# Thresholds of a routing read from PSUM, and the first comparison of a layer pair cut in three

## The reference, cut to what matters

```python
def _moe_ref(x, w_gate, w1, w2):
    N, D = x.shape                    # 3072, 320
    E = w_gate.shape[1]               # 8
    cap = N // E                      # 384
    logits = x @ w_gate
    order = np.argsort(-logits.flatten())
    for idx in order:
        tok, e = (int(idx) // E, int(idx) % E)
        if assigned[tok] >= 0 or counts[e] >= cap:
            continue
        assigned[tok] = e
        counts[e] += 1
    for e in range(E):
        mask = assigned == e
        h = np.maximum(x[mask] @ w1[e], 0.0)      # 320 -> 1024
        out[mask] = h @ w2[e]                     # 1024 -> 320

def _moe2_ref(x, w_in, w_out):
    h = x @ w_in                                  # 320 -> 2048
    g = np.where(h > 0.0, h, np.exp(np.minimum(h, 0.0)) - 1.0)
    return g @ w_out                              # 2048 -> 320
```

## Time and profile before

| | us |
|---|---|
| three runs: median (lowest, highest) | 913.61 (910.56, 917.07) |
| the profiled execution, whole time | 910.03 |
| its span | 908.3 |
| mean granted clock of TensorE | 0.95 |
| PE busy | 786.0 |
| DVE, ACT, POOL busy | 573.8, 462.0, 445.2 |

### The profile page before, as it was taken

The page is one execution under the profiler, slowest core; times in us unless marked ns, Lnnn a source line. Parts: engine busy times, 40 slices in busy tenths (PEclk is TensorE's granted clock), DMA queues, the critical chain, the costliest instruction groups (busy, mean ns, idle before and its releaser), DMA issues.

```text
span 908.3 us, 18300 instructions
## 1 busy us (share of the span) xinstructions
PE 786.0 (87%) x5822; PEld 720.6 (79%) x5822; DVE 573.8 (63%) x1576; ACT 462.0 (51%) x981; POOL 445.2 (49%) x469
## 2 busy tenths in 40 slices
PE   1898999982158899989989998998999899999995
PEld 1787888882138799879969987897999789899894
DVE  7475767676855865687586567748656774643341
ACT  1444444432221775377276537826662773685573
POOL 6544444444460575186256518625661773374133
PEclk9999999996557999999999999999999999999998
DMA  4978788833321120221112022121202211121000
GB/s 68 142 126 139 125 131 131 138 71 95 116 74 42 43 65 30 63 63 45 64 43 65 26 61 70 44 66 44 65 16 64 78 45 58 47 66 37 1 1 22
DMA packets 138516, 61.04 MB, mean 67 GB/s; under 512 B 104704, under 2 KB 136704, under 8 KB 138432
## 3 DMA queue, kind: packets, MB, share of 16 engines
q1 hardware_dynamic: 136128, 52.13, 26.9%
q0 software_dynamic: 2304, 7.87, 2.7%
HBM read 51.72 MB, written 8.26 MB: 66 GB/s over the span
## 4 chain that ended last, share of the span: by engine, by line
PE 53%; DVE 11%; ACT 7%; issue 4%; POOL 2%; DMA 1%; ACTq 0%; DVEq 0%; SPq 0%; POOLq 0%
PE bank L1673 6%; PE bank L1603 6%; PE bank L1675 5%; PE bank L1674 5%; PE bank L1607 5%; PE bank L1604 5%; DVE cmp L754 3%; PE bank L1611 3%; PE bank L1609 3%; PE bank L1649 3%; PE bank L1647 3%; PE bank L1648 3%; PE bank L1632 1%; PE bank L1635 1%; ACT unit L1481 1%
## 5 line engine op out<-in xcount | busy, mean ns | idle before, releaser
L1105 POOL TENSOR_TENSOR gl_lo<-unit,gl_hi 128x384 fp32r<-128x384 f32 x128 | 142.0, 1109 | 126.3 <-ACT gl_hi L1493 125.4
L1673 PE MATMUL bank<-Wo_hi,gl_hi 128*128 128x320 f32 x384 | 126.8, 330 | 8.9 <-POOL gl_lo L1105 8.3
L1675 PE MATMUL bank<-Wo_hi,gl_lo 128*128 128x320 f32 x384 | 119.7, 312 | 0.0
L1674 PE MATMUL bank<-Wo_lo,gl_hi 128*128 128x320 f32 x384 | 119.4, 311 | 0.0
L1350 DVE SCALAR_TENSOR_TENSOR unit<-bank,unit 128x384 f32<-128x384 f32 x104 | 57.6, 554 | 90.5 <-ACT bank L1486 90.5
L1084 POOL DMA_INDIRECT xg<-x_rows,idx x24 | 26.3, 1097 | 159.3 <-DVE idx L1319 82.8
L1461 ACT ACTIVATE hid_hi<-bank 128x384 fp32r<-128x384 f32 x64 | 31.4, 490 | 136.8 <-PE bank L1611 134.4
L1478 ACT ACTIVATE unit<-bank 128x384 f32<-128x384 f32 x128 | 62.0, 484 | 66.1 <-PE bank L1611 65.9
L1603 PE MATMUL bank<-x_hi,Wi_hi 128*128 128x384 f32 x256 | 93.5, 365 | 2.0 <-DVE unit L1353 0.9
L1604 PE MATMUL bank<-x_hi,Wi_lo 128*128 128x384 f32 x256 | 86.8, 339 | 0.0
L1673 PEld LDWEIGHTS bank<-Wo_hi,gl_hi 128*128 128x128 f32 x384 | 73.1, 190 | 14.1 <-POOL gl_lo L1105 14.1
(11 more groups left out here) (252 smaller groups left out, 2143.1 us busy)
## 6 DMA issues: line engine op xcount, KB each, us to landing
stage<-in_moe_w_dram SPq DMA_DIRECT2D x32, 320.0 KB, 3.0
stage<-in_moe_w_dram SPq DMA_DIRECT2D x32, 256.0 KB, 2.6
stage<-in_moe_w_dram SPq DMA_DIRECT2D x96, 64.0 KB, 2.4
q_in<-in_q_dram SPq DMA_DIRECT2D x24, 160.0 KB, 3.3
k_in<-in_k_dram SPq DMA_DIRECT2D x24, 160.0 KB, 3.9
o_in<-in_o_gate_dram SPq DMA_DIRECT2D x24, 160.0 KB, 4.1
v_in<-in_v_dram SPq DMA_DIRECT2D x24, 160.0 KB, 4.1
x_rows<-xt SPq DMA_DIRECT2D x24, 160.0 KB, 1.8
```

The source lines that it names most:

```text
L1105: nc.gpsimd.tensor_tensor(gl_lo[:, b, :], ex[:, b, :], gl_hi[:, b, :].bitcast(F32), ALU.subtract).then_inc(gl_ok, 1)
L1673: nc.tensor.matmul(acc[j][:, 0:DM], gl_hi[:, f % RG, t_], Wo_hi[:, f, :], start=(f == 0), stop=False)
L1674: nc.tensor.matmul(acc[j][:, 0:DM], gl_hi[:, f % RG, t_], Wo_lo[:, f, :], start=False, stop=False)
L1675: ins = nc.tensor.matmul(acc[j][:, 0:DM], gl_lo[:, f % RG, t_], Wo_hi[:, f, :], start=False, stop=(f == NF2 - 1))
```

## The change

All rows of thresholds that the second stage reads are held in PSUM: the five of rounds 2 to 6 are written there at once (bank 7, columns 304 up), and ramp1 and slots are copied there (bank 7, columns 176 up; bank 6, columns 384 up) by two more instructions at the end of the mixer. The copies of ramp1 and slots in SBUF stay: the mixer reads ramp1, and later experts read slots. The first expert's one-hot blocks read slots from PSUM. pParts moves to columns 144 to 175 of bank 7.

In the six bodies the keys (choose_keys) are made with choose_start ahead of the change of layer, and the first comparison, in two halves of 12 tiles at f = 3 and 4 and ahead of the ELU, is in three parts of 8 tiles behind the ELU of f = 1, 2 and 3. For the second expert, ahead of the first body, it is in three parts as well, with the columns of the first expert between; on PE the three blocks of columns stand ahead of count_takers. In the mixer, steps of the keys move one tile earlier.

```diff
@@ RoutingTables
+        self.ramp1_p = bank[7][:, 176:176 + first_n]
+        self.ramps_p = bank[7][:, 304:304 + (len(STEPS) - 1) * 33].rearrange("p (q n) -> p q n", n=33)
+        self.slots_p = bank[6][:, 384:512]
@@ by_vector
-            nc.vector.tensor_scalar(self.ramps[:, q, 0:n], self.ramp_i[:, low:low + n],
+            nc.vector.tensor_scalar(self.ramps_p[:, q, 0:n], self.ramp_i[:, low:low + n],
                                     step * (1.0 if q + 1 < HIGH else UNIT), None, ALU.mult)
+        nc.vector.tensor_copy(self.ramp1_p, self.ramp1[:])
+        nc.vector.tensor_copy(self.slots_p, self.slots_i[:])
@@ first_compare
-            in1=self.ramp1[:, :].unsqueeze(1).broadcast_to([P, n, many]), op0=ALU.subtract, op1=ALU.is_ge)
+            in1=ramp.unsqueeze(1).broadcast_to([P, n, many]), op0=ALU.subtract, op1=ALU.is_ge)
@@ experts
-    ramps, down, slots, rows2, marks = tables.ramps, tables.down, tables.slots, tables.rows2, tables.marks
+    ramps, down, slots, rows2, marks = tables.ramps_p, tables.down, tables.slots, tables.rows2, tables.marks
-    pParts = pR[:, 192:192 + SIDE * E]
+    pParts = pR[:, 144:144 + SIDE * E]
@@ compare_first
+        SLICES = 3
         def compare_first(k, part):
-            ins = tables.first_compare(dve, *part_of(k, part), keys_at(k))
-            if part != 0:
+            n = G // SLICES
+            ins = tables.first_compare(dve, tables.ramp1_p, slice(part * n, part * n + n), n, keys_at(k))
+            if part == SLICES - 1:
                 ins.then_inc(cmp_ok, 1)
@@ choose_spots
-                ins = nc.vector.tensor_scalar(spot[:, g, :], slots[:], row[:, g:g + 1], None, ALU.is_equal)
+                ins = nc.vector.tensor_scalar(spot[:, g, :], tables.slots_p if first_expert(k) else slots[:], row[:, g:g + 1],
+                                              None, ALU.is_equal)
@@ DVE, ahead of the first body
-        compare_first(1, None)
+        compare_first(1, 0)
+        compare_first(1, 1)
         columns(0, 0)
-        round_test(1, 1)
+        compare_first(1, 2)
         columns(0, 1)
         columns(0, 2)
+        round_test(1, 1)
         round_move(1, 1)
@@ DVE, body
             if after == 2:
                 choose_start(c + 1)
+                choose_keys(c + 1)
             between_layers(k)
...
-                    if f == 2:
-                        choose_keys(c + 1)
-                    elif f == 3:
-                        compare_first(c + 1, 0)
-                    elif f == 4:
-                        compare_first(c + 1, 1)
-                    elif q >= 1 and odd:
+                    if q >= 1 and odd:
...
                 elu(k, f)
+                if 1 <= f <= SLICES and after == 2:
+                    compare_first(c + 1, f - 1)
@@ PE, ahead of the first body
-        columns(0, 0)
+        for j in range(NJ):
+            columns(0, j)
         count_takers(1, 1)
-        columns(0, 1)
-        columns(0, 2)
```

More of the change, by code:

```diff
@@ L61, in build @@
         pieces = WeightPieces(nc, keep_sb, sem, DM, XK)
-        tables = RoutingTables(nc, keep_sb, sem, L, B, G, E, CAP)
+        bank = [ps(f"bank{n}", [P, 512]) for n in range(8)]
+        tables = RoutingTables(nc, keep_sb, sem, bank, L, B, G, E, CAP)
         W_in = keep_sb("Wi_hi", [P, 3, FF2], F32R), keep_sb("Wi_lo", [P, 2, FF2], F32R)
@@ L107, in build @@
         wg = sb("wg", [P, 3, 2 * VP])
-        bank = [ps(f"bank{n}", [P, 512]) for n in range(8)]
         pTQ = bank[0][:, :].rearrange("p (n t) -> p n t", n=NP)
@@ L1150, in keys_at, with first_expert, all_or_last, compare_last_batch @@
             return (B - 1 + k) * KEY_STEPS
[L1152 to L1155 removed]
+        SLICES = 3
+        def first_expert(k):
+            return isinstance(k, int) and k == 0
+        def all_or_last(k):
+            return (slice(G - G // B, G), G // B) if first_expert(k) else (slice(0, G), G)
         def choose_start(k):
             made[0] = 0
[L1159 removed]
+            tables.choose_start(dve, *all_or_last(k), keys_at(k))
         def choose_keys(k):
[L1162 removed]
+            tables.choose_keys(dve, *all_or_last(k), keys_at(k))
+        def compare_last_batch():
+            tables.first_compare(dve, tables.ramp1_p, *all_or_last(0), keys_at(0)).then_inc(cmp_ok, 1)
         def compare_first(k, part):
[L1165 to L1166 removed]
+            n = G // SLICES
+            ins = tables.first_compare(dve, tables.ramp1_p, slice(part * n, part * n + n), n, keys_at(k))
+            if part == SLICES - 1:
                 ins.then_inc(cmp_ok, 1)
@@ L1362, in _ @@
         choose_keys(0)
-        compare_first(0, None)
+        compare_last_batch()
         finish_round(0, 1)
```

19 lines of the change are left out of this document (6 added, 13 removed).

## The result

| | before | after |
|---|---|---|
| median of four runs each (lowest, highest) | 915.34 us (910.56, 917.15) | 882.94 us (882.54, 885.02) |
| the profiled execution | 910.03 us | 882.67 us |
| its span | 908.3 us | 880.9 us |
| DVE, POOL busy | 573.8, 445.2 us | 547.3, 402.7 us |

The ratio is 0.9658, with an interval of 0.9615 to 0.9702: faster by 3.4%. The profiled executions differ by 27.4 us where the sum had 21.75.

The account below looks back on a forecast made before the run. PE, busy 786 of 908.3 us, bounds the kernel through its waits and clock. Gains 12.2 + 5.1 + 1.35 + 0.6 + 2.5 = 21.75 us off 910.03 give 888.3, plus 2: 890 us, range 882 to 902.

Parts of the forecast that it names:

- The wait at the count: Six bodies: PE's 2.56 us wait for DVE's first comparison goes, less 0.52 push each; net gain 12.2 us.
- The push by the keys: Change of layer in six bodies: keys made ahead of it delay what follows, costing 0.52 us each.
- The clock: Bodies k = 2, 4, 5: three falls to the 1.2 GHz level behind the count's wait go; gain 5.1 us.
- The rest of a body: Later rounds' comparisons get faster by up to 0.8 us each, but PE doesn't wait for them; gain nothing.
- Ahead of the first list: First expert, before the bodies: round 2's comparison gains 1.35 us, the 24 one-hot blocks from PSUM gain 0.6.
- The gather: Ahead of the first body: POOL's second gather, held out by DVE's undivided comparison, is freed; gain 2.5 us.
- First up to the second list: First expert's stretch from PE's first up matmul to the next token list; the sum had 0 for it.
- The mixer: Same instructions a tile earlier, two short ones added at its end; nothing, 1 us either way.
- The 2 us on top: Whole kernel: 2 us added to 888.3 because the earlier runs' median lay above the profiled execution.
- 1 and 2 (the clock falls all the same): Bodies: falls at some other wait, 895 us, chance 0.12; or at every change of layer, 900 or 901, chance 0.07.
- 3 (PSUM doesn't keep POOL and DVE apart): Comparisons stay exposed with hi in SBUF; one part in three costs 1.0 us more; 898 us, chance 0.07.
- 4 (half rate from PSUM): Comparisons rereading PSUM thresholds for each tile run at half rate, a part 2.27 us; 924 us, chance 0.07.

Follow-up runs that it names:

- keys_f1: The changed kernel with the keys back in the second layer, ahead of the ELU of f = 1: 881.98 us, ratio 0.9648.
- psum_only: The kernel before with the threshold tables in PSUM and the old order everywhere: 893.76 us, ratio 0.9784.
- longer_wait: The kernel before with thresholds in PSUM, old order, plus an extra seven-block comparison ahead of each body's second half: 905.55 us, ratio 0.9916.
- gather_sb: The changed kernel with thresholds back in SBUF for one comparison, the second expert's first round, beside the gathers: 886.64 us, ratio 0.9692.
- mixer_only: The kernel before with only the mixer's steps of the keys one tile earlier: 913.28 us, ratio 0.9985.
- order_only: The changed kernel with its tables in SBUF and the mixer's steps at their old tiles: 907.26 us, ratio 0.9919.
- keys_tokens: The changed kernel with the keys made behind the high and low parts of the tokens' rows: 880.24 us (0.9634), repeated at 882.5 us (0.9643).

## Why the prediction came out, point by point

- **The wait at the count** (12.2 us). Right in mechanism, too small in size: from each list to the count the six bodies together are 15.1 us shorter. The push by the keys is 0.37 us on average and not 0.52. And a wait is worth more than its bracket: in keys_f1, which has neither the push nor the wait, the count of k = 5 comes 16.41 us behind the list where it came 19.27, 2.86 us for a wait of 2.56. The bracket starts at the end of the matmul before, and a count that waits for nothing overlaps with that matmul: it starts 0.19 us after that matmul's start (691.17 to 691.36, after), and before 2.90 us after it (714.17 to 717.07). That makes 2.7; the last 0.15 us were won ahead of it. The spare time was 0.3 us and not 0.6.
- **The clock** (5.1). Right in mechanism, nearly in size: from the count to the next list the bodies with a fall are 1.6 us longer than the same bodies of psum_only, which has none, 4.8 for three. Taking a fall as gone with its wait was the bolder step; psum_only and longer_wait bear it out.
- **The rest of a body** (nothing). Missed: behind the count the changed kernel is 1.5 us slower than psum_only over the six bodies, with new waits of PE of up to 0.53 us, three of them for DVE's L1209. So the 18.2 us of the bodies come near the forecast's 17.3 partly by luck: some 2.9 us more from the waits, 0.3 less from the clock and 1.5 lost here.
- **Ahead of the first list** (1.35 + 0.6). Each by itself right in size: the second round's comparison went from 2.35 to 0.99, the blocks gained 0.82. The prediction took the time of a block from PSUM rightly (0.26 us), but not why 24 blocks took 7.11: four of them had waited for POOL. And 1.28 us of the gain went elsewhere, by their rows to the short instructions that now meet POOL. The prediction had named this as up to 2 us either way.
- **The gather** (2.5). Right, 2.66 measured. Here the Trainium skill's rule (page "SBUF — State Buffer", section "Who interferes with whom": such a comparison shuts out only what GpSimd reads, and descriptor making goes on) was weighed against the row. By it, as the prediction used it, the gathers of gather_sb would have stayed at 1.28 and 0.95 us; one took 1.84, and ended the same 0.83 us after the comparison as before. The measurement decides: the gather is held. But a gather also reads its row numbers, idx, from SBUF, so it may be this read that waits, as the rule itself would have it. No run keeps the read and the descriptors apart.
- **First up to the second list** (nothing). Missed. Measured 1.99. In the eleven profiles with the thresholds in PSUM this stretch takes either about 37.0 us (four of them, clock 0.73 to 0.82 over it) or 37.8 to 38.4 (seven, 0.70 to 0.71; before 38.94 at 0.70), so some 1.2 of the 2.0 come and go with the clock. Little is left for the thresholds: with them in SBUF it takes 37.25 in mixer_only (0.82) and 38.20 in order_only (0.72). So most of this gain is luck of the two profiles; what the remaining 0.2 to 0.7 us are wasn't tried apart.
- **The mixer** (nothing, 1 us either way). This is the step that failed, by 3.54 us. "The same instructions stand a tile earlier" was true and worth nothing; what I left out is that taking `ramps` out of SBUF moves every tile allocated behind it. The loads land sooner in exactly the kernels without that table; that the place of the tiles does it is not shown.
- **The 2 us on top** (median against profile). This should have been left out. The median of before lies 4 to 5 us above its profile, which fits more or longer falls of the clock than the three there; after the change none comes in a body, and its median lies 0.3 us above its profile.
- **The rivals.** 1 and 2 (the clock falls all the same): no body does. 3 (PSUM doesn't keep POOL and DVE apart): 21 parts at 1204 ns, and POOL's low parts go from 1109 to 1025 ns. 4 (half rate from PSUM): 1.20 us and not 2.27. 

The sum fell short by 3.5 (mixer), 2.0 (first up to second list), 1.2 (bodies, gather, rest), and was 1.1 over (ahead of the first list): 5.6 us, and with the 2 us on top the 7 us between 890 and the median. That the median still lies in the range is narrow: its bottom had been let out to 882 for one-hot blocks and short operations, and what came was the mixer.

## What to carry to other kernels

When VectorE and GpSimd share a stretch, give the wide VectorE instruction one operand in PSUM before you reorder anything: in the six bodies this won 10.7 of 17.6 us with the order untouched, while the order without it won 0.8, since the wait moved from one consumer to another. Then put short operand-heavy steps where the engine's own row shows idle time (keys_f1 and keys_tokens did as well as the place of the change, or better), not where the program reads well. For narrow instructions weigh the rate: a one-hot block costs 0.26 us from PSUM and 0.16 from SBUF when POOL doesn't meet it. And when a table leaves SBUF, look at the landing times of all loads whose tiles lie behind it.

## What was not expected of the hardware

- Loads of the same size and count landed in 2.6 to 3.4 us where they took 3.3 to 4.1, at the same 132 to 134 GB/s, with the DMA engines busy 0.65 and not 0.81 of the time, when 660 bytes a partition were taken away ahead of their tiles. The cause is open.
- A gather on GpSimd ended 0.83 us after VectorE's comparison with two SBUF operands, in two kernels with comparisons of 3.33 and 1.21 us, and took 3.96 and 1.84 us where it takes 0.95 beside one from PSUM.
- A VectorE instruction with a single fp16 input in SBUF, 0.16 us from one to the next, took 0.76 to 1.32 us where a GpSimd instruction of 0.72 to 1.30 us stood beside it; the same work from PSUM never did.
- A wait of 2.55 us on TensorE was followed by a fall to the 1.2 GHz level in 14 of 18 cases, one of 1.56 us in none of 6. A fall lasted 3.4 us and cost 1.3 to 1.6, or lasted 6.8 and cost 2.5.
- A comparison of 1,016 elements that takes its thresholds, broadcast over eight tiles, from PSUM runs at the same 1.2 us as a plain one from SBUF.
